# Reordering the end and the middle of a pair in a fused recurrence and expert kernel

## The reference, cut to what matters

```python
def _attn_ref(r, k, v, w, a, b):          # 4 batches, 8 heads, 768 steps, 40 wide
    for t in range(S):
        y[:, :, t] = einsum('bhd,bhde->bhe', rt, state)
        Sa = einsum('bhde,bhe->bhd', state, at)
        state_decay = state * wt[:, :, None, :] - einsum('bhd,bhe->bhde', Sa, bt)
        state = state_decay + einsum('bhd,bhe->bhde', vt, kt)

def reference(...):
    x = attention output, 3072 tokens x 320
    x = (h - tanh(h)) @ w_out,  h = x @ w_in            # first MLP, 320 -> 2048 -> 320
    return sum over 4 experts of p_e * (relu(x @ w1[e]) @ w2[e])   # 320 -> 1024 -> 320
```

## Time and profile before

| what | value |
|---|---|
| median of 3 runs | 1586.53 us (1586.33 to 1588.02) |
| the profiled execution | 1586.63 us; its span in the trace 1584.8 us |
| PE busy | 1461.1 us, 92% |
| DVE busy | 829.0 us, 52% |
| ACT busy | 399.1 us, 25% |
| POOL busy | 367.3 us, 23% |
| chain that ended last | PE 81%, DVE 11%, DMA 2% |

### The profile page before, as it was taken

One profiled execution on the slowest core, in us unless ns is written; L12 is line 12 of the kernel. 1 busy time (PEld: TensorE's weight loads), 2 busy tenths in 40 slices (PEclk: granted clock), 3 DMA queues, 4 the chain that ended last, 5 costly groups with the idle time before them and its releaser, 6 DMA issues.

```text
span 1584.8 us, 37837 instructions
## 1 busy us (share of the span) xinstructions
PE 1461.1 (92%) x15888; PEld 1276.6 (81%) x15888; DVE 829.0 (52%) x1457; ACT 399.1 (25%) x814; POOL 367.3 (23%) x313
## 2 busy tenths in 40 slices
PE   3378789999999999999969999999999999999998
PEld 2266668878878977977958889999999999999997
DVE  7979768777777876944113343233323332333233
ACT  1022333333333333333323221111111111111111
POOL 6121545333332332312325302010020202020000
PEclk9977899999999999999989999999999999999999
DMA  8454683165066054030030320001010101000011
GB/s 220 132 145 117 183 210 102 45 169 135 5 184 155 6 155 123 1 85 24 1 108 1 90 67 29 8 0 36 0 37 0 36 0 36 0 0 0 0 50 50
DMA packets 87671, 108.71 MB, mean 69 GB/s; under 512 B 13630, under 2 KB 66686, under 8 KB 87542
## 3 DMA queue, kind: packets, MB, share of 16 engines
q1 hardware_dynamic: 86190, 106.17, 24.9%
q10 hardware_dynamic: 1352, 0.66, 0.2%
HBM read 75.94 MB, written 30.84 MB: 67 GB/s over the span
## 4 chain that ended last, share of the span: by engine, by line
PE 81%; DVE 11%; DMA 2%; issue 1%; POOL 1%; ACT 1%; SPq 1%; POOLq 0%; DVEq 0%; ACTq 0%
PE banks L1575 22%; PE banks L1585 21%; PE banks L875 10%; PE banks L884 9%; PE banks L644 2%; DVE tmp L1136 2%; DVE ld L1133 2%; PE banks L759 2%; DVE nvmak L1193 2%; PE banks L724 2%; PE banks L707 2%; PE banks L716 1%; PE banks L737 1%; PE banks L763 1%; PE banks L617 1%
## 5 line engine op out<-in xcount | busy, mean ns | idle before, releaser
L1575 PE MATMUL banks<-x2t,u 128*128 (+1 forms) x1536 | 376.7, 392 | 0.0
L1585 PE MATMUL banks<-u,hid 128*128 128x320 f32 x2304 | 362.5, 309 | 0.0
L1585 PEld LDWEIGHTS banks<-u,hid 128*128 128x128 f32 x2304 | 349.9, 188 | 13.1 <-issue 0.9
L1679 DVE SCALAR_TENSOR_TENSOR hid<-banks,hid 128x512 fp32r<-128x512 f32 x192 | 132.8, 692 | 404.5 <-ACT hid L1665 404.5
L1575 PEld LDWEIGHTS banks<-x2t,u 128*128 128x128 f32 x1536 | 282.4, 188 | 52.7
L1665 ACT ACTIVATE hid<-banks 128x512 fp32r<-128x512 f32 x192 | 114.9, 598 | 564.8 <-PE banks L1575 564.8
L875 PE MATMUL banks<-xt,wi 128*128 128x512 f32 x768 | 195.4, 398 | 14.6 <-POOL xt L1362 13.6
L884 PE MATMUL banks<-wo,hid 128*128 128x320 f32 x1152 | 183.5, 310 | 2.0 <-POOL hid L1367 1.6
L884 PEld LDWEIGHTS banks<-wo,hid 128*128 128x128 f32 x1152 | 174.5, 188 | 10.8 <-POOL hid L1367 3.8
L875 PEld LDWEIGHTS banks<-xt,wi 128*128 128x128 f32 x768 | 141.1, 190 | 43.3 <-POOL xt L1362 13.9
L1367 POOL TENSOR_TENSOR hid<-shared,hid 128x512 fp32r<-128x512 f32 x96 | 124.4, 1296 | 210.6 <-ACT hid L1048 210.6
(11 more groups left out here) (117 smaller groups left out, 1513.9 us busy)
## 6 DMA issues: line engine op xcount, KB each, us to landing
scaled_operands<-made SPq DMA_DIRECT2D x79, 192.4 KB
kb<-scaled_operands SPq DMA_DIRECT2D x46, 192.0 KB
made<-kbaw SPq DMA_DIRECT2D x38, 192.0 KB
made<-kbaw SPq DMA_DIRECT2D x41, 144.0 KB
raw<-w SPq DMA_DIRECT2D x8, 640.0 KB, 5.8
lam<-scaled_operands SPq DMA_DIRECT2D x46, 96.8 KB
at<-scaled_operands SPq DMA_DIRECT2D x46, 96.0 KB
raw<-w SPq DMA_DIRECT2D x8, 512.0 KB, 4.0
```

The source lines that it names most:

```text
L1575: mm = pe.matmul(self.p_up[f][:], self.u1[:, par, w, f * 128:(f + 1) * 128], self.xt[:, bass.ds(n, 1), x, :].rearrange("p o t -> p (o t)") ...
L1585: mm = pe.matmul(self.p_dn[t][:, 0:D], self.hid[:, f, h, t * 128:(t + 1) * 128], self.u2[:, par, w, f, :], start=(f == 0 and i == 0), stop ...
L1679: dve.scalar_tensor_tensor(out=ex.hid[:, f, 1, :], in0=ex.p_up[f][:], scalar=0.0, in1=ex.hid[:, f, 0, :].bitcast(F32), op0=ALU.max, op1=AL ...
```

## The change

It moves work within `pair(p)` of four engines; no operation is added or taken out.

- PE, end of a pair: `turn_answers(p)` moves from last place to the one ahead of `state_by_answers(p)`; `scores_low(p + 1)` follows, and `natural(p + 1, 1)` comes last. The waits for the shared bank are changed to match, ACT's copies too, and `diagonal` of a unit in an MLP and `turn_state` wait for the last natural copy.
- PE, middle of a pair: the second `diagonal` of a pair moves from behind `turn_state` to behind `result_by_answers(p - 1)`, and from pair 3 on `state_by_values(p)` moves from ahead of `answer(p, ., 1)` to behind the rests of block 2.
- DVE: from pair 3 on, the scans of the first unit move from ahead of `mask_ur` to behind sides 1, next to their reciprocal. The second half of the second unit's reciprocal moves from ahead of `save_low_rest` to behind sides 0 of the next pair; where `p % 4 == 3` it stays at the end, now behind `save_low_rest`.
- POOL: from pair 4 on, where `p % 4 < 3`, `decay_state(p)` comes ahead of the second unit's `scale`.

```diff
@@ diagonal, turn_state, turn_answers, natural (PE)
             if i in late_diagonals:
-                pe.wait_ge(ut_saved, (i - FIRST) // 2 + 1)
+                pe.wait_ge(kbn_saved[1], (i - FIRST) // 2 + 2)
...
-            if p:
-                pe.wait_ge(ut_saved, p)
-                if in_mlp(p - 1):
-                    pe.wait_ge(lt_saved, diagonals_before(p + 1))
-            else:
-                pe.wait_ge(kbn_saved[1], 1)
+            pe.wait_ge(kbn_saved[1], p + 1)
+            if p and in_mlp(p - 1):
+                pe.wait_ge(lt_saved, diagonals_before(p + 1))
...
             if p + 1 < NP:
-                pe.wait_ge(kbn_saved[1], p + 2)
+                pe.wait_ge(kbn_saved[0], p + 2)
...
-            if j:
-                pe.wait_ge(kbn_saved[0], p + 1)
+            if j and p:
+                pe.wait_ge(ut_saved, p)
+            elif j:
+                pe.wait_ge(kbn_saved[0], 1)
@@ pair (PE)
             turn_state(p)
-            for i in prepared[1:2]:
-                diagonal(i)
             right_side_rest(p, 0, 1)
             right_side_rest(p, 1, 1)
-            if p > 2:
-                state_by_values(p)
             answer(p, 0, 1)
             answer(p, 1, 1)
             if p and not after_mlp:
                 result_by_answers(p - 1)
+            for i in prepared[1:]:
+                diagonal(i)
             right_sides(p, 0, 2)
             right_sides(p, 1, 2)
             right_side_rest(p, 0, 2)
             right_side_rest(p, 1, 2)
+            if p > 2:
+                state_by_values(p)
             if more:
                 scores(p + 1, 0)
...
                 natural(p + 1, 0)
                 scores(p + 1, 1)
+            turn_answers(p)
             state_by_answers(p)
             if more:
+                scores_low(p + 1)
                 natural(p + 1, 1)
-                scores_low(p + 1)
-            turn_answers(p)
@@ pair (ACT): save_diagonal(prepared[1:]) behind save_answer(p, ., 1)
                 save_natural(p + 1, 0)
-                save_natural(p + 1, 1)
+            save_turned_answers(p)
             if p + 1 < NP:
                 save_low(p + 1)
-            save_turned_answers(p)
+                save_natural(p + 1, 1)
@@ pair (DVE)
+        def second_half_at_end(p):
+            return p > 1 and p % PPC == PPC - 1
...
-            for k in i[:1]:
-                scan(k, 0)
-                scan(k, 1)
-                if p < 2:
-                    invert_decay(k)
+            if p > 2 and prepared_in(p - 1) and not second_half_at_end(p - 1):
+                invert_half(prepared_in(p - 1)[1], 1)
+            if p < 2:
+                prepare(i[0])
             if finish:
                 mask_ur(p - 1)
...
             elif i:
-                invert_decay(i[0])
+                prepare(i[0])
...
             update_state(p)
-            if p > 1 and i:
-                invert_half(i[1], 1)
             if p + 1 < NP:
                 save_low_rest(p + 1)
+            if i and second_half_at_end(p):
+                invert_half(i[1], 1)
             some(4)
@@ pair (POOL)
-            for i in made_here:
+            first = 1 if p > 1 and p % PPC < PPC - 1 else len(made_here)
+            for i in made_here[:first]:
                 scale(i)
             decay_state(p)
+            for i in made_here[first:]:
+                scale(i)
```

More of the change, by code:

```diff
@@ L1016, in pair @@
             save_turned_state(p)
-            for i in prepared[1:]:
-                save_diagonal(i)
             for b in range(1, NB):
@@ L1021, in pair @@
                 save_answer(p, 1, b)
+                if b == 1:
+                    for i in prepared[1:]:
+                        save_diagonal(i)
                 if b == 2:
```

## The result

The changed kernel took 1597.4 us in the median (1591.9 to 1607.6, 14 runs), the kernel before 1588.1 us (1585.4 to 1596.3, 14 runs): a ratio of 1.0070, 95% interval 1.0056 to 1.0085. It is 9 to 11 us slower, where 5.3 were forecast. The profiled execution was its longest, 1607.64 us.

A forecast was written before the change was run, and what follows sets the result against it. PE was taken to bound the pairs, but not pairs 3 to 6. The terms -1.2 + 0.8 + 1.7 + 1.8 + 2.2 = +5.3 on 1586.63 gave 1591.9, median 1591.8 us; range 1587 to 1597.5.

The forecast's parts named there:

- the clock: Rival: changed order keeps TensorE at full clock in early stretches, 6 us back, 3 more if the earliest go; chance 0.08.
- Ten pairs with diagonals: Pairs 7, 9 to 11, 13 to 15, 17 to 19: earlier u-r scores leave 0.12 us each, 1.2 us gained.
- Pairs 21 to 23: PE's wait for turned answers goes, 0.12 gained, but `state_by_values` costs 0.58 in pairs 21 and 22: 0.8 us lost.
- Behind an MLP: Pairs 8, 12, 16, 20: moved `state_by_values` costs 0.58 each, less 0.65 filling idle time ahead of `scores`: 1.7 us lost.
- The start: Pair 4 starts 1.75 us later as DVE's inversion meets POOL's scaling; pair 6, 2.8 later less 0.6: 2.2 us lost.
- a step waits for one POOL instruction only: Rival at pair 4's start: a blocked DVE step gets in at POOL's next release, 0.8 us less, 1591.0; chance 0.10.
- The part of pair 6: POOL reaches the weight halves 2.8 us later, 1.05 of it pair 6's own; 0.6 taken back for later store issue.
- The raw load: Late scale delays SP's store and the load behind it; 5.8 us from POOL's end to landing: 1.8 us lost, nine pairs.
- the load as slow as in pair 10: Rival: the load takes 6.7 us from POOL's end in each of nine pairs, 9.0 lost, not 1.8: 1599; chance 0.12.

The follow-up runs named there:

- the last experiment: Changed order, raw load ahead of the store and `state_by_values` in its old place, both only from pair 8 on, against the kernel before, run again: 1587.0 us, 0.9993.
- the second profile: From the second set of runs of the changed kernel, nothing altered, against the kernel before: 1596.3 us (4 runs), 1.0080.

## Why the prediction was wrong in size

The direction was right and the changed kernel's steps went where they were said to go; the time came 5.6 us above the forecast, a hair inside the upper end. That it lies inside is luck: the upper end left out the clock and most of a slow load, and both came. Term by term:

- *Ten pairs with diagonals, -1.2.* Right, somewhat small: with the load out of the way they take 16.07 where they took 16.27 us, so 0.20 a pair and, taken for all ten (an estimate), 2.0. Both mechanisms are in the rows: no wait at L734, 0.38 before answers 1.
- *Pairs 21 to 23, +0.8.* Right: 2 x 0.35 = 0.7, and 15.22 us with `state_by_values` back.
- *Behind an MLP, +1.7.* Too large: 0.21 in pair 20, so 0.8 in all if the other three are like it. Of its 0.59 us in pair 20 the idle time ahead of `scores`, and an overlap of 0.07, took back 0.24. Another 0.14 came from ahead: the rests of block 2 start 2.09 us behind `turn_state` and not 2.23, so its old place had not been quite free.
- *The start, +2.2.* Pair 4 took 29.18 against 27.79 us, +1.4 for 1.75 said. With the order of pair 3's end alone put back it is 1.3, midway between the 1.75 and the 0.9 of the rival in which a step waits for one POOL instruction only, and the rows have one step of each kind. The part of pair 6 was mostly absorbed: pairs 3 to 7 are 0.6 and 1.7 us longer in the two profiles. That is less than one kernel differs from itself: the version of the last experiment took 94.6 and 90.8 us there in its two profiles.
- *The raw load, +1.8.* **This is the step that failed.** I took 5.8 us from POOL's end to the landing, because I took SP's queue to be idle and its transfers drained; in nine pairs it was 5.5 to 7.7, 6.6 in the mean, in the second profile, and 6.2 to 8.0 in the eight of the first in which the scans waited. At pair 10 the store alone was issued for 1.81 us. The nearest row said 6.7 and was right; the argument that shortened it was wrong. The kernel before had more such rows: in pair 9 (below) it was 7.9 us, from 324.47 to 332.33, and in pair 13 6.5. The term, said to be 1.8 us, measured 6.6: that much undoing this alone gave back in the profiles. The rival "the load as slow as in pair 10" (1599) was the better forecast, and I had given it 0.12; but its 9.0 us for the load are more than the 6.6 measured, and the clock, which it left out, made up for it.

```profile
323.79 0.68 POOL L1323 TENSOR_TENSOR made<-made 104x256 f32<-104x256 f32 x1
...
332.33 0.74 DVE L1088 TENSOR_TENSOR_SCAN made<-made 104x128 f32<-104x128 f32 x2 [1.23 <-DMA made<-kbaw]
```

- *What is not in the sum: the clock.* I had it only as a gain at the start. With the load term at 6.6, the others as measured make -2.0 + 0.7 + 0.8 + 6.6 + 1.2 (the middle of the start's two values) = 7.3 us, and the medians say 9.3 and 9.7. The rest is not told apart: the runs at a low mean clock add to it, and so may the start. The changed kernel's two low stretches followed its two longest idle times, and idle times of that length put into the kernel before brought such stretches behind two of the three. So a late transfer that cost 0.7 us in each of nine pairs came, in 5 of 14 runs of the first set and in none of 4 of the second, with some 12 us more; none of the 12 runs with the load first was that slow. One reading of this rival was off as well: from 88.8 to 218.5 us the kernel before has seven stretches at 0.50, not eight. The 24 us from 150 on are right.

What stays open: why the clock fell behind 1.42 us in one profile and not behind 1.48, 1.69 or 1.86 in others (over all profiles, from pair 7 to 23, it fell behind seven of the ten waits for right sides 3 of 1.4 to 2.2 us, and behind none of the three of 1.0 to 1.2); and why it fell as well in the version with the half reciprocal put back, where from 240 us on PE never idled longer than the 0.70 us that every version has ahead of the first answers behind an MLP. It has two waits in each pair (0.59 and 0.32) where the kernel before has one of 0.48, which was not tried by itself. The early stretches at 1.2 GHz differ from run to run with the code unchanged: the profiled execution of the changed kernel reached pair 4 at 172.9 us, the second set's at 168.4.

## What to carry to other kernels

When an instruction that releases a store moves later, follow the queue: every load behind that store moves with it, and its time from the release to the landing is to be read from the row of the same load, not argued down. Let loads go ahead of stores that wait. And where the matrix engine is the bound, look at the granted clock behind every idle time: three of 1.5 to 2.2 us in full stretches cost two and a half times their length in one kernel here, and nearly four times in another.

## What was not expected of the hardware

- 5.6 us of idle time of PE in three pieces of 1.5 to 2.2 us cost 14.1 us in the median, with 0.50 granted for 6.8 and 17.1 us behind two of them.
- A pause of PE of 1.30 us without any releaser in the profile was followed at once by such a stretch (470.7 to 474.2 us).
- The clock also fell right behind waits of 0.58 and 0.59 us, three times in the profile of the version with the half reciprocal put back.
- The same two stores were issued by SP in 0.78 to 0.81 us in six pairs of the changed kernel's first profile and in 1.78 to 1.81 us in pairs 10, 11 and 17. The same three pairs were the slowest in the second profile (1.49, 1.20, 1.57). Why stays open.
- A VectorE step of 0.2 us waited through two GpSimd instructions, 2.01 us in all, and another (1.29 us) through one only.
